# Moving steps in a hand-written software pipeline: key-value products beside the outputs, fillers in larger groups, roots and loads at other places

## The reference

```
for t in range(S):                                # stage 1, per batch and head
    new_re = ar * S_re - ai * S_im                # a_n = a * min(|a|, 0.999) / (|a| + 1e-6)
    new_im = ar * S_im + ai * S_re
    kv = einsum('bhd,bhe->bhde', k[:, :, t], v[:, :, t])
    S_re, S_im = new_re + kv, new_im
    y[:, :, t] = einsum('bhd,bhde->bhe', q[:, :, t], S_re)
x = y as 3072 tokens of width 384
xn = x / sqrt(mean(x * x) + 1e-6) * rms_g         # stage 2, inner width 1536
x = silu(xn @ w_gate) * (xn @ w_val) @ w_out
h = maximum(x @ w1[expert], 0); out = gate * (h @ w2[expert])   # stage 3, expert by argmax
```

## Time and profile before

| | us |
|---|---|
| median of 3 runs | 1306.32 (1303.97 to 1306.84) |
| the profiled execution | 1303.45 |
| its span | 1301.7 |
| PE busy | 1203.5 (92%) |
| DVE busy | 766.8 (59%) |
| ACT busy | 600.7 (46%) |
| POOL busy | 366.4 (28%) |

### The profile page before, as it was taken

One profiled execution on the slowest core, in us unless ns is written; L12 is line 12 of the kernel. 1 busy time (PEld: TensorE's weight loads), 2 busy tenths in 40 slices (PEclk: granted clock), 3 DMA queues, 4 the chain that ended last, 5 costly groups with the idle time before them and its releaser, 6 DMA issues. The chain is left out here.

```text
span 1301.7 us, 46434 instructions
## 1 busy us (share of the span) xinstructions
PE 1203.5 (92%) x20081; PEld 1041.7 (80%) x20081; DVE 766.8 (59%) x1549; ACT 600.7 (46%) x1293; POOL 366.4 (28%) x361
## 2 busy tenths in 40 slices
PE   1788999999999999999999999999978999999996
PEld 0556787879687887878687887878857999999996
DVE  5696847485767658484667557263117555555553
ACT  3646354545546554646455554434222344333442
POOL 8506051323333150413333150200003122222221
PEclk9899999999999999999999999999997999999998
DMA  7142011111202020111111020000005634333410
GB/s 206 26 123 59 7 39 40 39 40 33 45 15 57 9 58 20 38 40 39 39 30 42 9 45 10 15 15 3 13 13 161 209 127 143 132 134 131 137 37 30
DMA packets 151845, 78.36 MB, mean 60 GB/s; under 512 B 130715, under 2 KB 144571, under 8 KB 151664
## 3 DMA queue, kind: packets, MB, share of 16 engines
q1 hardware_dynamic: 143264, 59.04, 17.0%
q0 software_dynamic: 4384, 11.88, 3.1%
q10 hardware_dynamic: 4016, 4.73, 1.0%
HBM read 66.15 MB, written 11.06 MB: 59 GB/s over the span
## 5 line engine op out<-in xcount | busy, mean ns | idle before, releaser
L887 PE MATMUL pO<-wo_sb,hid 128*128 128x384 f32 x576 | 206.9, 496 | 4.0 <-issue 2.8
L572 DVE TENSOR_TENSOR hid<-silu,pGV 128x256 f32<-128x256 f32 x144 | 60.0, 417 | 177.2 <-ACT silu L711 177.2
L887 PEld LDWEIGHTS pO<-wo_sb,hid 128*128 128x128 f32 x576 | 102.6, 191 | 58.6 <-issue 5.2
L873 PE MATMUL pGV<-xT_hi,wg_hi 128*128 128x256 f32 x432 | 139.4, 323 | 6.1 <-DVE hid L572 6.1
L711 ACT ACTIVATE silu<-pGV 128x256 f32<-128x256 f32 x144 | 55.4, 385 | 181.1 <-PE pGV L875 178.9
L1198 ACT ACTIVATE h_hi<-pH 128x256 fp32r<-128x256 f32 x128 | 49.1, 385 | 164.9 <-PE pH L1143 164.9
L875 PE MATMUL pGV<-xT_hi,wg_lo 128*128 128x256 f32 x432 | 122.4, 283 | 1.0 <-issue 1.0
L874 PE MATMUL pGV<-xT_lo,wg_hi 128*128 128x256 f32 x432 | 122.0, 282 | 0.0
L873 PE MATMUL pGV<-xT_hi,wv_hi 128*128 128x256 f32 x432 | 121.5, 281 | 0.0
L874 PE MATMUL pGV<-xT_lo,wv_hi 128*128 128x256 f32 x432 | 121.5, 281 | 0.0
L875 PE MATMUL pGV<-xT_hi,wv_lo 128*128 128x256 f32 x432 | 121.2, 281 | 0.0
(11 more groups left out here) (213 smaller groups left out, 3043.9 us busy)
## 6 DMA issues: line engine op xcount, KB each, us to landing
w_sb<-in_moe_w SPq DMA_DIRECT2D x18, 1536.0 KB, 10.5
re<-in_a_re SPq DMA_DIRECT2D x24, 192.0 KB, 2.9
im<-in_a_im SPq DMA_DIRECT2D x24, 192.0 KB, 3.7
qin<-in_q SPq DMA_DIRECT2D x24, 192.0 KB, 2.8
kin<-in_k SPq DMA_DIRECT2D x24, 192.0 KB, 3.6
vin<-in_v SPq DMA_DIRECT2D x24, 192.0 KB, 3.3
routed_rows<-x ACTq DMA_DIRECT2D x24, 192.0 KB, 2.0
wo_sb<-in_moe_w_out SPq DMA_DIRECT2D x1, 2304.0 KB, 9.5
```

The source lines that it names most:

```text
L572: w.tensor_tensor(hid[:, f, :], act_g[f % 2], pGV[f % 2][:, TOKS:2 * TOKS], ALU.mult).then_inc(sm["h_ready"], 1)
L873: mm.matmul(to, hi, x_hi[:, kk, :], start=(kk == 0), stop=False)
L887: ins = mm.matmul(pO[:, 0:HD], hid[:, f, s_ * P:(s_ + 1) * P], wo_sb[:, f, :], start=(f == 0), stop=(f == NF - 1))
```

## The change

Seven things are changed together.

1. `STEPS` is another list. Outputs of chunk 0, its key-value products and, later, key-value products and outputs of chunk 1 stand side by side; gates and outs stand in pairs and threes between the levels; `logits` follows level 4.
2. The key-value products are a step of their own (`products`) and go into pG of their chunk instead of pM. They no longer wait for the copy of the outputs out of pM. Waits for that copy move to the outputs and to `phase`.
3. `roots` belongs to `sq`: it stands at the end of pass i, ahead of the copy of the last output, for the pair that pass i+1 treats.
4. The squares of the outputs are written to x2 instead of a tile shared with the phases.
5. SP's loads: the values, queries and keys for a pass are issued when its first two turns are done, and the decays for two passes ahead after the sums. Before, each was issued when the last reader of its buffer had finished. SP's loop is written out.
6. Lead-in: two fills of 128x1024 go from POOL to DVE, eight mask copies from POOL to ACT, PE and DVE no longer wait for all constants, and the load of w_out (2304 KB) is issued after those for pass 1.
7. The fillers become one per missing `out` and two per missing `gate`; before, two per `out` and three (five gates) or one (seven gates).

```diff
-BUSY_TURNS, BUSY_LEVELS, BUSY_END = 2, 3, 1
+BUSY_TURNS, BUSY_LEVELS = 1, 2
...
-    ("lev", "output", 0), ("lev", "output", 1), ("glu", "gate", 7),
-    ("lev", "state", 0), ("glu", "gate", 8), ("sq", "squares", 0), ("sq", "squares", 1), ("glu", "gate", 9),
-    ("lev", "output", 2), ("lev", "output", 3), ("glu", "gate", 10), ("sq", "abs", 0), ("sq", "abs", 1), ("glu", "gate", 11),
+    ("lev", "output", 0), ("lev", "output", 1), ("lev", "products", 0), ("glu", "gate", 9), ("lev", "state", 0), ("sq", "squares", 0),
+    ("sq", "squares", 1), ("glu", "gate", 10), ("sq", "abs", 0), ("sq", "abs", 1), ("glu", "gate", 11), ("sq", "roots", 0), ("sq", "roots", 1),
+    ("lev", "products", 1), ("lev", "output", 2), ("lev", "output", 3),
     ("lev", "state", 1),
 ]
...
-                            sp.wait_ge(sm["t_ready"], n0 - U + u + 1)
...
-                            sp.wait_ge(sm["kv_ready"], n0 + u + 1)
...
+                            sp.wait_ge(sm["tp_ready"], i * TA + TA + 2)
+                            values(i)
+                        if 0 < i < NP - 1:
+
+                            sp.wait_ge(sm["kcs_ready"], n0 + U + CREDIT)
+                            queries_and_keys(i + 1)
+                        if i < NP - 2:
+
+                            sp.wait_ge(sm["ima_ready"], n0 + 2 * U)
+                            sp.wait_ge(sm["absre_ready"], n0 + 2 * U)
+                            decays(i + 2)
...
-                    for u in range(U):
-                        done(g.memset(A[u][:, :, :], 0.0))
...
+                    for u in range(U):
+                        w.memset(A[u][:, :, :], 0.0).then_inc(sm["a_cleared"], 1)
...
                                 if "pre" in stages:
-                                    act.wait_ge(sm["thp_ready"], np_ + U)
-                                s.activation(thr[0][:, :, :].rearrange("p h d -> p (h d)"), xs[u], ACT.Square, accum_out=ssq[:, u:u + 1]).then_inc(sm["ssq_ready"], 1)
+                                s.activation(x2[u][:, :], xs[u], ACT.Square, accum_out=ssq[:, u:u + 1]).then_inc(sm["ssq_ready"], 1)
...
-                            elif step == "state":
+                            elif step == "products":
                                 u = x
                                 pe.wait_ge(sm["evac_done"], i * TA + CREDIT + TF + 2 + 2 * u)
-
-                                pe.wait_ge(sm["x_ready"], n0 + u + 1 + ONE)
...
-                                        ins = mm.matmul(pM[at, h * D:(h + 1) * D], KTM[u][:, h, at], v_t[u][:, h, :], start=True, stop=True)
+                                        ins = mm.matmul(pG[u][at, h * D:(h + 1) * D], KTM[u][:, h, at], v_t[u][:, h, :], start=True, stop=True)
```

More of the change, by code:

```diff
@@ new lines @@
+    ("glu", "norm", 0), ("lev", "turn", 0), ("lev", "turn", 1), ("fin", "out", 0),
+    ("lev", "turn", 2), ("lev", "turn", 3), ("pre", "sums", 0), ("pre", "sums", 1), ("fin", "out", 1),
+    ("lev", "turn", 4), ("lev", "turn", 5), ("glu", "scale", 0), ("pre", "recip", 0), ("lev", "first", 0), ("fin", "out", 2),
+    ("lev", "turn", 6), ("lev", "turn", 7), ("wts", "split", 0), ("pre", "recip", 1), ("fin", "out", 3),
+    ("lev", "turn", 8), ("lev", "turn", 9), ("pre", "quotients", 0), ("fin", "out", 4),
@@ new lines @@
+    ("lev", "turn", 10), ("lev", "turn", 11), ("lev", "first", 1), ("pre", "quotients", 1), ("wts", "split", 1), ("fin", "out", 5),
+    ("fin", "square", 0), ("pre", "tangent", 0), ("pre", "tangent", 1),
+    ("lev", "level", 0), ("fin", "out", 6), ("fin", "out", 7), ("fin", "out", 8), ("glu", "turn_in", 0),
+    ("lev", "level", 1), ("pre", "double", 0), ("pre", "double", 1), ("fin", "out", 9), ("fin", "out", 10), ("fin", "out", 11),
+    ("wts", "split", 2), ("lev", "level", 2), ("fin", "square", 1), ("glu", "gate", 0), ("glu", "gate", 1),
@@ new lines @@
+    ("lev", "level", 3), ("pre", "angle", 0), ("fin", "route", 0), ("glu", "gate", 2), ("glu", "gate", 3),
+    ("wts", "split", 3), ("lev", "level", 4), ("fin", "logits", 0), ("pre", "angle", 1), ("glu", "gate", 4), ("glu", "gate", 5),
+    ("lev", "level", 5), ("pre", "phase", 0), ("glu", "gate", 6),
+    ("wts", "split", 4), ("lev", "level", 6), ("pre", "phase", 1), ("pre", "own", 0), ("glu", "gate", 7),
+    ("lev", "turn_back", 0), ("pre", "rotate", 0), ("pre", "own", 1), ("glu", "gate", 8),
@@ L107 @@
 FIRST_STEPS = [("pre", step, u) for step, u in (
-    ("roots", 0), ("roots", 1), ("sums", 0), ("sums", 1), ("recip", 0), ("recip", 1),
+    ("masks", 0), ("sums", 0), ("sums", 1), ("recip", 0), ("recip", 1),
     ("quotients", 0), ("tangent", 0), ("angle", 0), ("double", 0),
@@ L262, in load, with decays @@
                                      ).then_inc(loaded[u], 16)
[L264 to L265 removed]
+                    def decays(i):
                         for u in range(U):
[L267 to L272 removed]
@@ L313, in _ @@
                         sp.dma_start(landing[n % 2], (w_gate, w_val)[n // KC][n % KC * P:(n % KC + 1) * P, :]).then_inc(staged[n % 2], 16)
-                    batch(0, range(1, NJ), False)
-                    with sp.Fori(1, B - 1) as b:
-                        batch(b, range(NJ), False)
-                    batch(B - 1, range(NJ), True)
+                    for i in range(NP):
+                        n0 = i * U
+                        if i > 0:
+                            sp.wait_ge(sm["tp_ready"], i * TA + TA + 2)
[7 more added lines that the diff above has]
+                            decays(i + 2)
                 @block.gpsimd
@@ L356, in _ @@
                                              pattern=[[2 * L, nb], [0, L]], channel_multiplier=-1))
-                    for j in range(NBLOCK):
-                        rows_ = slice(j * BLOCK, (j + 1) * BLOCK)
-                        done(g.tensor_copy(level_mask[rows_, :, :], wide_mask[rows_, :, j * ODD:(j + 1) * ODD]))
-                        done(g.tensor_copy(own_mask[rows_, :], ident[rows_, rows_]))
                     assert step == n_consts
@@ L749, in body @@
                             if stage not in stages:
-                                if "lev" in stages and "fin" not in stages and step in ("gate", "out"):
-                                    busy(BUSY_TURNS if step == "out" else BUSY_LEVELS if x < 5 else BUSY_END)
+                                if "lev" in stages and step in ("gate", "out"):
+                                    busy(BUSY_TURNS if step == "out" else BUSY_LEVELS)
                                 continue
@@ L910, in body @@
                                 ins.then_inc(sm["lg_ready"], 1)
-                    pipeline(pe, body, True)
+                    pipeline(pe, body)
         x = ExitStack()
```

104 lines of the change are left out of this document (42 added, 62 removed).

## The result

The changed kernel takes 1315.81 us (median of 15 runs, 1309.38 to 1322.58), the kernel before 1305.0 in the same session (15 runs, 1301.83 to 1310.87): 1.008 times as long, 95% interval 1.0062 to 1.0097. I had forecast 1300.0, a gain. The profiled execution took 1315.95 us, its span is 1314.2, 12.5 more than before. I read the windows first, for the same five stretches as the earlier trace rows.

The account below looks back on a forecast made before the run. PE was taken to set the pace in passes 2 to 9, busy 561.05 of 580.70 us. Terms of -8, +8, -3 and -2 summed to -5 us: 1298.5, or 1300 with 1.5 added; range 1273 to 1317.

Parts of the forecast that it names:

- The end of a pass: Passes 2 to 9: PE waits for ACT's first evacuation before the third turn, DVE's squares colliding with POOL; +2.7 us a pass.
- The clock: Passes 2 to 9: old clock dips go, -0.4 us a pass; new dips behind every second gap, +0.85.
- Waits that go: Passes 2 to 9: grouped gates and outs remove PE's waits, -1.8 us a pass; gate 10's wait for gate 8's product, +0.4.
- Tile blocks joined: Passes 2 to 9: 9 narrow blocks instead of 12 mean fewer changes of tiling mode, -0.8 us a pass.
- Passes 0 and 1: First two passes: weight pieces moved, a wait for a copy gone, twelve fillers fewer; about -8 us, between -15 and 0.
- The weight pieces: Pass 0: three pieces leave the levels, -5.4 us; two go into the turns, +2, one in front of the state, +2.
- The outputs' wait for the copy: Pass 0: the outputs no longer wait for the copy out of pM, -2 us.
- Pass 10: Pass 10, without squares and roots: fewer blocks, waits and clock dips against a gap of about 1.2 us; -3 us.
- Pass 11: Pass 11: -0.8 us for joined blocks and about 1.2 of waits gone; -2 us.
- Lead-in: Before pass 0: mask copies leave POOL, two fills come to DVE, gain and loss about equal; 0, between -2 and +2 us.
- Stage 3 "is not touched": The stretch from 974 us on: claimed untouched by the change, with no term in the sum.
- the slower one (clock, 1320): Rival, chance 0.17: PE at 1.2 GHz for 6.8 us after each pass's end, +20 us on the forecast, 1320.
- It does not do what it says: Rival, chance 0.10: unexplained stalls stay and DVE's waits move elsewhere, so waits gain 0.8 a pass, not 1.8; 1309 us.

Follow-up runs that it names:

- x2: The changed kernel with logits and products moved behind gates, away from other narrow blocks: 1300.05 us, ratio 0.9956 to the kernel before.
- x4: The changed kernel with more fillers in passes 0 and 1, two per out and three per gate: 1326.67 us, ratio 1.0162 to the kernel before.
- x8: The kernel before with only gates 1 to 8 and out 11 moved forward: 1306.15 us, ratio 1.0004.
- x14: x6 with the low halves of the six weight pieces ahead of levels 1 to 6 again: 1290.32 us, ratio 0.9879 to the kernel before.
- x6: The changed kernel with gate 8 moved into the pass's end, logits and chunk 1's products apart from narrow blocks, two lead-in fills on POOL: 1291.44 us.
- x15: x6 with one filler instead of two for each gate of passes 0 and 1: 1294.91 us against 1291.44.
- x16: x6 with two fills of a single unused column added on DVE in the lead-in: 1296.67 us.
- x7: The kernel before with only the key-value products put into the level sums' bank, at their old places: 1313.02 us, ratio 1.0065.
- x12: The changed kernel once more, unedited, for a second profile: 1317.29 us in one run.
- x11: x6 with logits, key-value products and outputs all made of whole tiles: 1358.68 us, ratio 1.0414 to the kernel before.

## Why the prediction was wrong

My sum was -5 us on the profiled execution, and +12.5 came. The 1315.8 us lie inside the wide range that I gave, 1273 to 1317, at its upper edge; that is no merit, since I had forecast a gain and a loss came, and half of it, the 6.4 us behind the router, had no term in the sum.

**The end of a pass** was right as a mechanism: the walk down the four queues gave the collision (L442 2.0 us), the order on ACT and the releaser. The wait was over-sized: 2.7 us a pass, measured 11.6 / 8 = 1.45, between 0.17 and 2.38. The clock: +0.45 net a pass forecast, measured (17.1 - 6.8) / 2 / 8 = +0.64; the size is near by luck, since only two of eight gaps had it and the stalls, which I had not counted, brought the rest.

**Waits that go** is the step that failed in the passes. I forecast -1.8 and +0.4 a pass. All waits of PE except the one for the evacuation were 19.0 us in passes 2 to 9 before and 17.3 after: -0.2 a pass. DVE's went, as said, but I had counted the unexplained stalls (issue) as something that wider spacing removes. Instead they doubled, 8.5 to 16.8 us. They stand where a step of 256 rows ends behind a fast stretch, and the joining made such stretches more common (3.5% to 12.4% of the rows); x2, with the blocks apart, has 2.4 us of them. How much of the doubling is the place alone, x4 tells: 8.3 us with the same list. I had even named "in which PE eats most instructions", and drew the wrong sign.

**Tile blocks joined**, -0.8, was right in size. What is left of +1.19 a pass after the three terms above is 1.19 - 1.45 - 0.64 + 0.2 = -0.7, and PE's busy time says the same: 559.72 - 561.05 = -1.3 us, less the 5.1 that the clock added, is -6.4, -0.8 a pass. My derivation of it was weaker than the result: the lone gate of 2.32 us stands behind a turn-back, which uses the whole array, so it has a narrow block on one side only. From blocks with narrow work on both sides, two gates take 4.45 us and three 6.61, two outs 2.78 and three 4.07; that makes 0.13 and 0.20 us for each interruption. x8 shows that the gain isn't to be had alone: about 0 for the kernel. That passes 2 to 9 came out at +9.5 for my +8 is two errors that cancel: the wait 1.2 a pass too large, the stalls 1.2 too small.

**Passes 0 and 1**, -8: measured -1.1, failed by the sign that I had set. The weight pieces are worth 0, not -1.4 (x14 against x6). The outputs' wait for the copy, -2 in the sum, was 1.6 us and did go, but their wait for DVE's state grew from 2.0 to 4.6. The sum counted twelve fillers less, in pass 1, for 4 us; in fact 22 went, ten of them in pass 0. They came with 13.6 us more at half clock (27.3 for 13.7), and x15 shows the same exchange. "I count nothing more" for the clock there was the mistake. In pass 0 PE also waits 10.7 us for the evacuation (7.4 before), and in pass 1, where I had looked for no gap, 3.9.

**Pass 10**, -3: -3.3. **Pass 11**, -2: -0.1; nothing isolates why.

**Lead-in**, 0: the fills on DVE cost some 2.4 us at the start (33.7 to 35.2 us in eight profiles, 31.6 to 33.4 in the nine with the fills on POOL), and what else changed in the lead-in gives part of it back (before: 34.0); no run takes the masks alone. The net is +1.0, inside the bounds of -2 to +2.

**Stage 3 "is not touched"** failed too: +6.4, a term that I had put at nothing. The code was not touched, but the place of its instructions in DVE's stream was; x16, with two tiny instructions more, has 304.9 us there against 298.2 in x6.

Of the rivals, the slower one (clock, 1320) was nearest in time but wrong in cause: the clock cost 0.64 a pass more than before, not 3.0 (3.4 less the old 0.4). "It does not do what it says" had the nearest cause, stalls that stay, at too low a price: they grew.

## What to carry to other kernels

Joining blocks of short products is paid for in instruction supply: look in the waits of PE for "issue" at the shortest tiles, number PE's rows to see whether such waits stand 256 rows or a multiple apart, and put long products between the blocks. When a step moves forward, walk ACT, DVE and POOL to the next thing that PE needs from them, and put one independent block of PE's there: that single gate was worth 11 us of the kernel. Compare untouched stretches too before a sum is closed; two tiny instructions elsewhere can move them.

## What the runs showed of the hardware

PE stopped up to 2.8 us in the middle of a block of 32-column tiles with nothing awaited (302.1 us of the changed kernel). All 147 such waits of 0.5 us or more in passes 2 to 9 of twenty profiles stand 256 rows of its queue, or a multiple of that, apart. The Trainium skill (Runtime: NRT & Kernel Launch, Instruction fetch mechanics) describes how engines fetch their instructions ahead, in blocks of 256. The traces agree on the 256. The same section calls the cost at a block's end mostly hidden; behind fast stretches here it was 0.5 to 2.8 us, and the measurement decides.

In passes 2 to 10 the granted clock fell to half at waits of PE of 1.25 (x7) to 2.75 us (x12), not at all of them, and in x11 behind 10 us without any idle time, in a row of whole-tile products with 48 columns. Such a whole product came every 0.22 us, four short ones took 0.11.

L442 on DVE, 0.35 us alone, took 2.0 beside a POOL operation on 128x768 (seven of eight passes). Two one-column fills on DVE at 10 us made the stretch behind 985 us longer by 6.8 us (x16 against x6).
